# First rows of sums in place for both batches, the third slot's constant rows copied by DMA, and gate splits one a step

## What is computed

```python
scores = scale * np.matmul(q, k.transpose(0, 1, 3, 2))
s_pos = np.maximum(s, 0.0)
cum = np.cumsum(s_pos, axis=-1)
bias = -(cum[:, :, :, None] - cum[:, :, None, :])
scores = np.where(causal, -1000000000.0, scores + np.minimum(bias, 0.0))
attn = softmax(scores)                      # written out in the reference
x = np.matmul(attn, v)                      # to (1152 tokens, 512)
x = top-2 of 8 experts, relu(x @ w1[e]) @ w2[e], gates x @ w_gate, x @ w_noise
x = all 8 experts, shares from 8 Sinkhorn steps over exp(x @ moe2_w_gate)
```

## Time and profile before

| | |
|---|---|
| median of three runs | 1203.97 us (1203.75 to 1205.89) |
| profiled execution | 1204.84 us, of which the span of its instructions is 1203.1 us |
| PE busy | 1188.2 us, 99% |
| DVE, ACT, Pool busy | 697.3, 426.4, 254.8 us |
| granted clock of PE, mean | 0.993 |

### The profile page before, as it was taken

The page is one execution under the profiler, slowest core; times in us unless marked ns, Lnnn a source line. Parts: engine busy times, 40 slices in busy tenths (PEclk is TensorE's granted clock), DMA queues, the critical chain, the costliest instruction groups (busy, mean ns, idle before and its releaser), DMA issues.

```text
span 1203.1 us, 20068 instructions
## 1 busy us (share of the span) xinstructions
PE 1188.2 (99%) x7085; PEld 1062.0 (88%) x7085; DVE 697.3 (58%) x1584; ACT 426.4 (35%) x918; POOL 254.8 (21%) x303
## 2 busy tenths in 40 slices
PE   8999999999999999999999999999999999999998
PEld 6999888888888888889889899899899898898997
DVE  6664775554444451657566575575574675665753
ACT  7675344444344241224123232242241241332320
POOL 8767111111111456201001011011010010110110
PEclk9998999999999999999999999999999999999999
DMA  7770654444455420013120220210211201202102
GB/s 179 182 173 4 246 179 153 155 150 153 180 180 203 161 61 1 1 36 106 36 71 6 64 70 0 70 40 30 70 35 35 70 24 46 70 0 70 35 1 78
DMA packets 40230, 102.81 MB, mean 85 GB/s; under 512 B 4750, under 2 KB 23694, under 8 KB 38010
## 3 DMA queue, kind: packets, MB, share of 16 engines
q1 hardware_dynamic: 33722, 85.70, 22.7%
q0 software_dynamic: 3360, 11.01, 3.0%
q10 hardware_dynamic: 3104, 5.54, 1.4%
HBM read 87.82 MB, written 10.30 MB: 82 GB/s over the span
## 4 chain that ended last, share of the span: by engine, by line
PE 95%; DVE 2%; ACT 1%; DMA 1%; issue 1%; POOL 0%; DVEq 0%; POOLq 0%
PE bank L1164 10%; PE bank L1163 10%; PE bank L1162 9%; PE bank L1118 9%; PE bank L1116 9%; PE bank L1117 9%; PE bank L940 5%; PE bank L942 5%; PE bank L941 5%; PE bank L922 5%; PE bank L924 4%; PE bank L923 4%; PE bank L847 3%; PE bank L828 1%; PE bank L792 1%; PE bank L829 1%
## 5 line engine op out<-in xcount | busy, mean ns | idle before, releaser
L1164 PE MATMUL bank<-part2h,partl 128*128 128x512 f32 x504 | 198.6, 394 | 0.0
L1163 PE MATMUL bank<-part2l,parth 128*128 128x512 f32 x504 | 197.6, 392 | 0.0
L761 POOL TENSOR_TENSOR part2l<-raw_part,part2h 128x512 fp32r<-128x512 f32 x56 | 72.4, 1293 | 589.9 <-ACT part2h L1414 589.9
L1162 PE MATMUL bank<-part2h,parth 128*128 128x512 f32 x504 | 195.7, 388 | 0.0
L1886 DVE SCALAR_TENSOR_TENSOR x_sb<-bank,share_now,x_sb 128x512 f32<-128x512 f32 x126 | 94.1, 747 | 159.5 <-PE bank L1164 159.5
L1118 PE MATMUL bank<-x_forms,forml 128*128 128x288 f32 x448 | 132.1, 295 | 0.0
L1116 PE MATMUL bank<-x_forms,formh 128*128 128x288 f32 x448 | 131.9, 294 | 0.0
L1117 PE MATMUL bank<-x_forms,formh 128*128 128x288 f32 x448 | 131.8, 294 | 0.0
L1565 DVE SCALAR_TENSOR_TENSOR hl<-bank,hh 128x336 fp32r<-128x336 f32 (+1 forms) x88 | 45.7, 519 | 131.5 <-ACT hh L1291 131.3
L922 PE MATMUL bank<-xTh,w1h 128*128 128x336 f32 (+1 forms) x352 | 115.9, 329 | 0.7 <-DVE xTl L1545 0.5
L923 PE MATMUL bank<-xTl,w1h 128*128 128x336 f32 (+1 forms) x352 | 113.9, 324 | 0.0
(11 more groups left out here) (244 smaller groups left out, 2464.2 us busy)
## 6 DMA issues: line engine op xcount, KB each, us to landing
raw<-in_w SPq DMA_DIRECT2D x15, 2048.0 KB, 7.7
raw_part<-in_w1b SPq DMA_DIRECT2D x14, 1024.0 KB, 6.0
raw_part<-in_w2b SPq DMA_DIRECT2D x14, 1024.0 KB, 6.1
k_raw<-in_kT SPq DMA_DIRECT2D x16, 288.0 KB, 5.3
y_dram<-x_sb ACTq DMA_DIRECT2D x16, 256.0 KB, 4.4
q_raw<-in_qT SPq DMA_DIRECT2D x8, 288.0 KB, 5.0
q_two<-w2l SPq DMA_DIRECT2D x8, 288.0 KB, 5.8
x_dram<-x_sb SPq DMA_DIRECT2D x1, 2304.0 KB, 9.2
```

The source lines that it names most:

```text
L1162: pe.matmul(dst, parth[:, l, ts], part2h[:, l, :], start=(l == 0), stop=False)
L1163: pe.matmul(dst, parth[:, l, ts], part2l[:, l, :], start=False, stop=False)
L1164: mm = pe.matmul(dst, partl[:, l, ts], part2h[:, l, :], start=False, stop=(l == FL - 1))
```

## The change

The first rows of sums are now made in place for both batches of head 0: s's first row of each batch is loaded to 32 rows of its own (the second by ACT), the low parts are formed for all rows at once with a vector row_low (1 where a row is to hold the low part) and a row_sign, and ACT copies batch 1's two rows. Head 1's rows go by four small DMAs, without DRAM. The scaling of s moves from DVE to ACT. The constant rows of slot 1 of q_top are Pool's, and those of slot 2 of k_top and q_top are copied by four DMAs of 32 rows each, for which SP waits ahead of load_cum(2). The fillers get narrower. The copy that presets rinv moves to step -1. The six gate splits run one a step, at k = 57, 58, 59, 62, 63 and 64. WARM_UPS goes from 3 to 5. The diff, cut to its core (left out: new semaphores' declarations, three linked operations of one column that make row_low and row_sign, the body of split_gates, which is the same six operations):

```diff
...
-            sp.dma_start(cum_s[0:FIRST_ROWS, :], s[0:1, :].to_broadcast([FIRST_ROWS, S])).then_inc(s_loaded, 16)
+            sp.dma_start(cum_s[0:BATCH_ROWS, :], s[0:1, :].to_broadcast([BATCH_ROWS, S])).then_inc(s_loaded, 16)
...
             def load_cum(h):
                 w = h % HEADS_RING
-                if h < HEADS_RING:
-                    sp.wait_ge(aug_ready, 2 + h)
-                if h == 1:
+                if h == 2:
                     sp.wait_ge(cum_stored, 32)
...
-            def second_cum(row, part):
-                sp.dma_start(k_top[0][row:row + 1, S:N].bitcast(F32), part[FIRST_ROWS + 1:FIRST_ROWS + 2, :].bitcast(F32)).then_inc(cum_loaded[0], 16)
+            def second_head_cum(row, part):
+                for b in range(B):
+                    at = FIRST_ROWS + B + b
+                    sp.dma_start(k_top[1][row:row + 1, b * S:(b + 1) * S].bitcast(F32), part[at:at + 1, :].bitcast(F32)).then_inc(cum_loaded[1], 16)
+
+            def copy_rows(to, constant):
+                sp.dma_start(to, constant).then_inc(rows_copied, 16)
...
             sp.wait_ge(cum_high, 1)
-            sp.wait_ge(aug_ready, 2)
-            second_cum(HD, cum_h)
+            sp.wait_ge(rows_filled, 3)
+            second_head_cum(HD, cum_h)
             sp.dma_start(cum_rows[:, 0, :], cum_h[CUM_ROWS, :].bitcast(F32)).then_inc(cum_stored, 16)
             sp.wait_ge(cum_low, 1)
-            second_cum(HD + 1, cum_l)
+            second_head_cum(HD + 1, cum_l)
             sp.dma_start(cum_rows[:, 1, :], cum_l[CUM_ROWS, :].bitcast(F32)).then_inc(cum_stored, 16)
+            double_q(0)
             load_v(0)
-            double_q(0)
-            load_cum(1)
             double_q(1)
             sp.wait_ge(low, LOWS)
             load_raw(2)
+            load_v(1)
+            sp.wait_ge(q_rows_ready, 2)
+            copy_rows(k_top[2][HD:ROWS_ROUGH, :].bitcast(F32), k_top[1][ROWS_ROUGH:P, :].bitcast(F32))
+            copy_rows(k_top[2][ROWS_ROUGH:P, :].bitcast(F32), k_top[1][ROWS_ROUGH:P, :].bitcast(F32))
+            copy_rows(q_top[2][HD:ROWS_ROUGH, :].bitcast(F32), q_top[1][HD:ROWS_ROUGH, :].bitcast(F32))
+            copy_rows(q_top[2][ROWS_ROUGH:P, :].rearrange("p (b s) -> p b s", b=B).bitcast(F32),
+                      zeros_g[0:P - ROWS_ROUGH, :].unsqueeze(1).to_broadcast([P - ROWS_ROUGH, B, S]))
+            load_v(2)
+            sp.wait_ge(rows_copied, 64)
             load_cum(2)
-            load_v(1)
-            load_v(2)
...
-            for w in range(HEADS_RING):
-                pool.memset(k_top[w][HD:P, :].bitcast(F32), 1.0).then_inc(aug_ready, 1)
-            pool.memset(q_top[2][HD:P, :].bitcast(F32), 0.0).then_inc(q_rows_clear, 1)
+            for w in range(2):
+                pool.memset(k_top[w][HD:P, :].bitcast(F32), 1.0).then_inc(rows_filled, 1)
+            pool.memset(q_top[1][HD:P, :].bitcast(F32), 0.0).then_inc(rows_filled, 1)
+            pool.wait_ge(rows_filled, 4)
+            pool.wait_ge(q_rows_ready, 1)
+            pool.memset(q_top[1][HD:HD + 2, :].bitcast(F32), 1.0).then_inc(q_rows_ready, 1)
...
-                if k == LAST_ROWS_AT:
-                    pool.wait_ge(q_rows_clear, 1)
-                    pool.wait_ge(q_rows_ready, 2)
-                    pool.memset(q_top[2][HD:HD + 2, :].bitcast(F32), 1.0).then_inc(q_rows_ready, 1)
...
-                        pe.wait_ge(cum_loaded[w], 16 * (h // HEADS_RING + (1 if w else 2)))
+                        pe.wait_ge(cum_loaded[w], 16 * (h // HEADS_RING + (0, 4, 1)[w]))
...
-                    if h < HEADS_RING:
+                    if h < 2:
                         pe.wait_ge(q_rows_ready, h + 1)
+                    if h == 2:
+                        pe.wait_ge(rows_copied, 64)
                 if h == 0 and k == STEPS:
                     pe.wait_ge(q_high, 1)
-                    pe.wait_ge(cum_loaded[0], 32)
...
-                keep_warm(BANK)
+                keep_warm(BANK // 2)
...
-                    keep_warm(BANK // 2 if k < -SCORES_AHEAD else P)
+                    keep_warm(P)
...
+            act.dma_start(cum_s[BATCH_ROWS:FIRST_ROWS, :], s[1:2, :].to_broadcast([BATCH_ROWS, S])).then_inc(s_loaded, 16)
             act.dma_start(cum_s[CUM_ROWS, :], s).then_inc(s_loaded, 16)
             act.wait_ge(const_ready, 5)
             act.copy(ident_r[:], ident[:]).then_inc(ident_rounded, 1)
+            act.wait_ge(s_loaded, 48)
+            act.activation(cum_p[0:CUM_END, :], cum_s[0:CUM_END, :], ACT.Relu, scale=SQRT_D).then_inc(s_positive, 1)
...
-            for w in range(2):
-                act.activation(q_top[w][HD:P, 0:S], causal[HD:P, 0:S], ACT.Relu, bias=row_ones[HD:P, 0:1], scale=0.0)
-                act.activation(q_top[w][HD:P, S:N], causal[HD:P, 0:S], ACT.Relu, bias=row_ones[HD:P, 0:1], scale=0.0).then_inc(q_rows_ready, 1)
+            act.activation(q_top[0][HD:P, 0:S], causal[HD:P, 0:S], ACT.Relu, bias=row_ones[HD:P, 0:1], scale=0.0)
+            act.activation(q_top[0][HD:P, S:N], causal[HD:P, 0:S], ACT.Relu, bias=row_ones[HD:P, 0:1], scale=0.0).then_inc(q_rows_ready, 1)
...
             act.copy(k_two[0][:, 0:S], k_raw[:, 0, 0:S]).then_inc(first_high, 1)
+            act.wait_ge(cum_low, 1)
+            act.copy(k_top[0][HD:HD + 2, S:N], cum_l[BATCH_ROWS:BATCH_ROWS + 2, :].bitcast(F32))
             act.copy(k_top[0][0:HD, S:N], k_raw[0:HD, 0, S:N])
...
-            link(v.tensor_copy(rinv[:].rearrange("p a b -> p (a b)"), ones[:, 0:2 * STEPS]))
-            v.wait_ge(s_loaded, 32)
-            link(v.tensor_scalar(cum_p[0:CUM_END, :], cum_s[0:CUM_END, :], 0.0, SQRT_D, ALU.max, ALU.mult))
+            v.wait_ge(s_positive, 1)
             v.tensor_tensor_scan(cum_s[0:CUM_END, :], cum_p[0:CUM_END, :], zeros_g[0:CUM_END, :], 0.0, ALU.add, ALU.add).then_inc(cum_summed, 1)
             v.wait_ge(cum_summed, 1)
-            link(v.tensor_scalar(cum_p[0:2, :], cum_s[0:2, :], ident[0:2, 1:2], None, ALU.mult))
+            link(v.tensor_scalar(cum_p[0:CUM_END, :], cum_s[0:CUM_END, :], row_low[0:CUM_END, 0:1], None, ALU.mult))
...
-            v.tensor_tensor(cum_l[CUM_ROWS, :], cum_s[CUM_ROWS, :], cum_h[CUM_ROWS, :].bitcast(F32), ALU.subtract).then_inc(cum_low, 1)
+            v.scalar_tensor_tensor(out=cum_l[0:CUM_END, :], in0=cum_h[0:CUM_END, :].bitcast(F32), scalar=row_sign[0:CUM_END, 0:1],
+                                   in1=cum_p[0:CUM_END, :], op0=ALU.mult, op1=ALU.add).then_inc(cum_low, 1)
...
-            def split_gates():
-                v.wait_ge(gates_loaded, 48)
...
+            def split_gates(step):
+                which, part = divmod(step, 3)
...
+                if k == -1:
+                    link(v.tensor_copy(rinv[:].rearrange("p a b -> p (a b)"), ones[:, 0:2 * STEPS]))
+                if k in GATES_AT:
+                    split_gates(GATES_AT.index(k))
...
```

More of the change, by code:

```diff
@@ L156, in build @@
         row_sign = sb("row_sign", [P, 1], where=attn)
+        row_low = sb("row_low", [P, 1], where=attn)
         attn.close()
@@ L204, in build @@
         s_loaded = sem("s_loaded")
+        s_positive = sem("s_positive")
+        rows_copied = sem("rows_copied")
         cum_summed = sem("cum_summed")
@@ L210, in build @@
         ident_rounded = sem("ident_rounded")
-        q_rows_clear = sem("q_rows_clear")
         q_rows_ready = sem("q_rows_ready")
@@ L224, in build @@
         const_ready = sem("const_ready")
-        aug_ready = sem("aug_ready")
+        rows_filled = sem("rows_filled")
         rough_ready = sem("rough_ready")
@@ L371, in build @@
         ROUGH_AHEAD, SCORES_AHEAD = 13, 4
-        WARM_UPS = 3
+        WARM_UPS = 5
         WARM_TOP2, WARM_RANKS, WARM_GATHER, WARM_BACK = 27, 4, 6, 29
@@ L383, in build @@
         HIGH_AHEAD, LOW_AHEAD = 19, 14
-        W1_LOW_AT, EARLY_AT, GATES_AT = ALL - 4 * DC, ALL - ST, 60
+        W1_LOW_AT, EARLY_AT, GATES_AT = ALL - 4 * DC, ALL - ST, (57, 58, 59, 62, 63, 64)
         EARLY = ST
-        FIRST_ROWS = 32
+        BATCH_ROWS = 32
+        FIRST_ROWS = B * BATCH_ROWS
         CUM_END = FIRST_ROWS + G
         CUM_ROWS = slice(FIRST_ROWS, CUM_END)
-        SECOND_LATER, LAST_ROWS_AT = 2, 4
+        SECOND_LATER = 2
         FIRST_LOWS = (0, 1, 4, 5, 2, 3, 6, 7)
@@ L597, in _ @@
             pool.memset(causal[:], 0.0).then_inc(const_ready, 1)
-            pool.memset(aug[:].bitcast(F32), 0.0).then_inc(aug_ready, 1)
+            pool.memset(aug[:].bitcast(F32), 0.0).then_inc(rows_filled, 1)
             pool.memset(v_sb[:, :, :, 0:1], 1.0).then_inc(const_ready, 1)
@@ L1516, in token_low @@
                                 xTh[:, :, ts].bitcast(F32), ALU.subtract).then_inc(st.xTl_ready, 1)
-            def split_gates():
-                v.wait_ge(gates_loaded, 48)
-                for which, (cn, c0, g0) in enumerate(((2 * E, 0, 0), (E, 2 * E, 4 * E))):
-                    high, low = gate_w[:, :, g0:g0 + cn], gate_w[:, :, g0 + cn:g0 + 2 * cn]
+            def split_gates(step):
+                which, part = divmod(step, 3)
```

(17 more changed lines are left out.)

6 lines of the change are left out of this document (4 added, 2 removed).

## The result

| | kernel before | changed kernel |
|---|---|---|
| median of 22 runs each | 1202.78 us | 1206.42 us |
| range | 1200.21 to 1207.75 | 1204.57 to 1217.56 |
| profiled execution (span) | 1204.84 (1203.1) | 1208.39 (1206.7) |

The ratio is 1.0040, with a 95% interval of 1.0025 to 1.0054: 3.0 to 6.5 us slower. The forecast was 1203.2, 0.8 us faster.

What follows compares the result with a forecast made beforehand. PE, busy 99%, bounds the kernel: -1.1 idle, -4.8 old fall, +1.1 later head 2, +4.0 new fall make -0.8 from 1204.84, so 1204.0; less 0.87 for the median, 1203.2 us. Range 1197.2 to 1207.5.

Steps and rivals of the forecast that it cites:

- What bounds the kernel: Whole kernel: PE busy 99%; time comes only from PE standing still, half clock or filler matmuls; attention is where to look.
- Gate splits: Attention near 97 us: splits run one a step no longer delay PE, so 1.09 us of idle go.
- The fall near 100: Attention, 99.94 to 110.18 us: PE's half clock behind the idle goes with it, saving 4.8 us.
- The fill: Kernel start: scan about 1.1 us earlier, first rough tile 0.5 to 1.0 us earlier, first scores about 0.9.
- The give-back: Kernel start: DVE's multiplication meeting Pool's memset, and ACT's extra copy (about 0.6 us), take back some of the earlier scan.
- Rows of the third slot: Head 2's start: SP waits for four row copies, so its first rough tile starts 1.1 us later, near 28.9.
- rival B: Head 2's start: SP's wait is long, tile 3.9 us later plus a 4.8 us fall: +2.8, 1206.8 us; chance 0.17.
- The fall behind it: Behind head 2's late first tile: about 2.1 us of PE idle brings a new clock fall costing 4.0 us.
- A: Head 2's stall is short or keeps the clock: 1197.2 with the fill's 0.9 us kept, or 1199.2; chance 0.24.
- C: Clock still falls near 100 (+4.0, 1208.0), or thinner warm-ups leave half clock past first scores (up to +2); together 0.09.

Runs made afterwards that it cites:

- v_later: Changed kernel with SP issuing v(2) only after the row copies, their wait, head 2's cumulative rows and second K copy: 1205.11 us, ratio 1.0026 to the kernel before.
- head_only: Changed kernel with third-slot constant rows written by VectorE instead of DMA copies, and gate splits in one block: 1198.54 us against 1203.30 of the kernel before, ratio 0.9972.
- before_filled: Kernel before with five more filler matmuls of 128 columns ahead of the 74th rough tile: 1201.20 us against 1200.25, ratio 1.0001.

## Why the prediction was wrong, point by point

**What bounds the kernel, and where to look.** Right: what the change does, it does through PE's idle and PE's clock in attention. The range held the time; the sign was wrong.

**Gate splits.** The mechanism is right. The idle of 1.09 us is gone; each split stands between two maxima. Two of them, and the maximum behind the first:

```profile
97.30 0.58 DVE L1544 TENSOR_TENSOR gate_w<-gates,gate_w 128x64 fp32r<-128x64 f32 x1
98.05 0.56 DVE L1493 CUSTOM_DVE_ANT_0 unused<-bank,causal 128x384 fp32r<-128x384 f32 x1 [0.17 <-DVE gate_w L1544]
...
105.43 0.63 DVE L1546 TENSOR_TENSOR fold<-ident 16x8 f32<-16x8 f32 x1
```

**The fall near 100, -4.8. This is the step that failed.** The size is right for an execution that has it (4.5 to 4.7 in the table). Wrong is that I counted it in full. "Against the profiled execution's own 1204.84" I took off a fall that this execution had and most have not, and then went over to the median by subtracting 0.87 us. A trace with the fall and a median without it can't be joined by a constant. One trace and three runs could not show how often it comes. The term was worth -1.6 at most: 3.2 us or more of the 4.4 between forecast (-0.8) and measurement (+3.6).

**The fill.** Forecast: first rough tile at 8.1 to 8.6, scan near 4.7. Measured: 7.93 and 4.61. The give-back did not come. From the timelines of DVE and POOL:

```profile
4.61 1.35 DVE L1472 TENSOR_TENSOR_SCAN cum_s<-cum_p,zeros_g 80x576 f32<-80x576 f32 x1 [0.94 <-ACT cum_p L1247]
6.00 0.52 DVE L1474 TENSOR_SCALAR cum_p<-cum_s,row_low 80x576 f32<-80x576 f32 x1
```

```profile
6.16 1.35 POOL L626 MEMSET w2l<- 2x1152 f32 x1 [0.68 <-ACT w2l L1251]
```

The multiplication ran in 0.52 us beside the memset; the memset took 1.35 instead of 1.05. If anyone paid for that meeting, it was POOL.

**Rows of the third slot.** Forecast: copies in at 25.2, double_k(2) at 25.7, the tile at 28.9 (+1.1), 2.1 us of idle. Measured: 26.37, 26.74, 30.11 (+2.27), 3.46. This term is the other 1.2 us. The rate was right: in v_later the bytes were all but through at 24.0, with SP 0.5 us ahead, where I had 24.7, so 32 rows do not move at a share of 128 rows' rate, and rival B's 3.9 us are out. Two terms I had at nothing: the tail of the last copy, 1.2 us, and v(2) beside it, 0.3 to 0.7.

**The fall behind it, +4.0.** Forecast within 4 us, 10.2 us long; measured at 27.9, 10.2 us, costing 6.12 - 2.27 = 3.85. But the sum treats it like the one near 100, and they are not alike. In all 23 executions of the changed kernel the mean clock is 0.996 or less, as a fall of 10.2 us leaves it, and both traces have the fall, so this stall brings one as good as always, and it can last 30.7 us and cost 13.4. That is also the changed kernel's range to 1217.56.

**The sum again**, with what the runs showed: -1.1 idle, -1.6 at most for the fall near 100 (a third of 4.8), +2.3 tile, +3.85 fall: +3.4, or more. Measured: +3.6 by the medians, +4.8 by the means, 3.0 to 6.5 by the ratio. A third of a cost belongs into a mean; on a median a fall that comes in a third of the executions can weigh less, and the changed kernel's few long falls show mostly in the mean. In the same way, a straight line through the 35 executions of the kernel before on the first chip gives 1.04 us for each 0.001 of mean clock, and 1200.0 at 1.000; through the changed kernel's 22, 0.96 us and 1201.0. The medians of the clock are 0.997 and 0.994. So about 1 us is steady work and waiting, and about 3 are clock.

**The rivals.** A did not happen; the head start it speaks of is real, 1.2 us instead of 0.9, and shows as soon as the copies go. B named the right wait and its sign, with the rate for a reason, which was wrong. Its rule, that the sign turns at a delay of 1.9 us, rested on the -5.9 as well; with -2.7 at most any delay with a fall of 4 us is slower. C did not happen in the changed kernel's two traces. Its half clock past the first scores was seen once with the thin warm-ups, in head_only, but also once with the wide ones (9.7 to 13.1 us in before_filled), so it does not speak against them.

**Still open**: why the same idle of 1.1 us brings a fall in one execution and none in the next, how often it does so exactly, and what sets the length of one (3.4, 6.8, 10.2, 13.7 and 30.7 us were seen).

## What to carry to other kernels

Before a stall's clock fall goes into a sum, look at several executions: one trace says that it can happen, the spread of the mean clock over the runs says how often, and in the mean only that share of it is worth anything. Ahead of a DMA on the critical chain, a full queue had no cheap place for four small copies in the four orders tried; VectorE's memsets of 1 us, in gaps where it mostly waits anyway, left PE 0.4 us of idle and no fall. And a wait for a transfer can end well after the queue has gone quiet: here by 1.6 us, of which 1.2 are the last eight packets.

## What the runs showed of the hardware

- An idle of 1.06 to 1.14 us of TensorE in attention was followed by 10.2, 0, 13.7, 0 and 0 us at 1.2 GHz in five traces of three kernels that share it.
- Idles of 2.1 to 3.8 us between 24 and 30 us came with a fall that began during them or within 0.5 us in every trace that has them (6 of 6), and with none where filler matmuls took their place (1 of 1). Size is not all: the idle of 2.4 us ahead of the warm-ups and the one of 1.7 to 1.9 us near 430 (five traces) brought none.
- A fall behind the same stall lasted 10.2 us in one execution and 30.7 in another, with TensorE busy for 30.00 of 30.00 us in it.
- The DMA queue was nearly empty (share 0.08, then 0.01) for 1.6 us before four copies of 144 KB had counted: 1.2 us for eight packets of 2304 bytes, 0.45 us from the last of them to the count.
- A VectorE memset of 1152 columns took 1.02 us on two rows as on 64.
